# Banded attention and two gated layers on one core: a head pair's scores and products with v issued in one run per tile of tokens

## The reference

```python
scores = q @ k.T / sqrt(D)                     # float32, per batch and head
mask = (rel >= 0) & (rel < 64)                 # rel = row - column
attn = softmax(where(mask, scores, -1e9))      # sum + 1e-9 below the line
x = (attn @ v) as (2304, 512)
x = max(x @ w1, x @ w2, x @ w3) @ w_out        # 512 -> 768 -> 512
h = x @ w_in                                   # 512 -> 2048
g = where(h >= 1, h, where(h <= -1, 0, (h + 1)**2 / 4))
out = g @ w_out2                               # 2048 -> 512
```

## Time and profile before

| what | us |
|---|---|
| three runs: median, lowest, highest | 772.2, 771.97, 772.84 |
| the profiled execution: its time | 771.65 |
| its span in the trace | 769.9 |
| TensorE busy | 752.1 (98%) |
| VectorE, ScalarE, GpSimd busy | 330.5, 334.0, 312.8 |
| DMA: bytes moved, mean | 46.18 MB, 60 GB/s |

### The profile page before, as it was taken

How to read it: one execution, slowest core, us unless ns; L and a number is a source line. 1 busy time by engine, 2 the same in 40 slices (tenths; PEclk the granted TensorE clock), 3 DMA queues, 4 the chain that set the end, 5 groups by cost and what they waited for, 6 DMA issues and landing times.

```text
span 769.9 us, 12651 instructions
## 1 busy us (share of the span) xinstructions
PE 752.1 (98%) x4680; PEld 655.0 (85%) x4680; DVE 330.5 (43%) x759; ACT 334.0 (43%) x809; POOL 312.8 (41%) x242
## 2 busy tenths in 40 slices
PE   5999999999999999999999899999999999999998
PEld 3888777777787888999999798899899899899886
DVE  3363233233223202261334663565766375367334
ACT  5662533542353120354253563365555355345332
POOL 4760111210111070185235873384777266257321
PEclk9999999999999999999999999999999999999999
DMA  8633232132110210020001110001120002201302
GB/s 311 234 103 95 62 96 80 34 101 71 43 43 14 83 56 1 0 80 29 0 1 56 55 47 36 1 29 55 55 83 28 1 1 90 76 0 55 110 1 83
DMA packets 24040, 46.18 MB, mean 60 GB/s; under 512 B 2224, under 2 KB 3632, under 8 KB 23984
## 3 DMA queue, kind: packets, MB, share of 16 engines
q1 hardware_dynamic: 23984, 45.43, 17.7%
HBM read 37.55 MB, written 7.86 MB: 59 GB/s over the span
## 4 chain that ended last, share of the span: by engine, by line
PE 94%; DVE 2%; POOL 1%; ACT 1%; DMA 1%; issue 1%; SPq 0%; DVEq 0%
PE wide L523 30%; PE wide L595 25%; PE bank L575 23%; PE wide L548 8%; PE bank L509 3%; PE wide L487 3%; PE bank L498 2%; POOL w3s L990 1%; DVE part_in L938 0%; DMA q<-q_dram 0%; DMA raw<-w_dram 0%; ACT prob L617 0%; DVE h1s L812 0%; POOL prob L998 0%; ACT pT L631 0%
## 5 line engine op out<-in xcount | busy, mean ns | idle before, releaser
L523 PE MATMUL wide<-xT,w 128*128 128x512 f32 (+1 forms) x1080 | 240.5, 376 | 0.0
L523 PEld LDWEIGHTS wide<-xT,w 128*128 128x128 f32 x1080 | 186.6, 190 | 36.6 <-issue 3.4
L595 PE MATMUL wide<-w4s,gT 128*128 128x512 f32 x864 | 210.1, 392 | 0.0
L575 PE MATMUL bank<-yT,w3s 128*128 128x384 f32 x1008 | 188.2, 337 | 2.2 <-POOL w3s L990 2.2
L595 PEld LDWEIGHTS wide<-w4s,gT 128*128 128x128 f32 x864 | 161.1, 188 | 31.2
L575 PEld LDWEIGHTS bank<-yT,w3s 128*128 128x128 f32 x1008 | 178.2, 188 | 8.4 <-POOL w3s L990 2.6
L990 POOL TENSOR_TENSOR gT<-g,gT 128x384 fp32r<-128x384 f32 x96 | 105.4, 1109 | 178.4 <-ACT gT L612 178.4
L998 POOL TENSOR_TENSOR prob<-prob,row_inv 128x512 f32<-128x512 f32 x36 | 38.2, 1060 | 186.7 <-DVE row_inv L829 186.7
L735 ACT ACTIVATE g_sq<-g_sq,half 128x384 f32<-128x384 f32 x96 | 58.0, 615 | 126.9 <-DVE g_sq L925 126.6
L913 DVE TENSOR_TENSOR pu<-bank,pu 128x384 f32<-128x384 f32 x72 | 40.1, 557 | 141.5 <-PE bank L575 136.5
L843 DVE TENSOR_TENSOR h<-wide,h 128x512 f32<-128x512 f32 (+1 forms) x60 | 38.2, 637 | 104.0 <-PE wide L523 103.4
(11 more groups left out here) (52 smaller groups left out, 538.7 us busy)
## 6 DMA issues: line engine op xcount, KB each, us to landing
v<-v_dram SPq DMA_DIRECT2D x36, 256.0 KB, 2.6
raw<-w_dram SPq DMA_DIRECT2D x16, 512.0 KB, 3.5
k<-k_dram SPq DMA_DIRECT2D x16, 288.0 KB, 3.2
h<-moe_w_dram SPq DMA_DIRECT2D x12, 384.0 KB, 8.0
q<-q_dram SPq DMA_DIRECT2D x16, 256.0 KB, 3.8
part_dram<-o_sb SPq DMA_DIRECT2D x12, 256.0 KB, 2.1
part_in<-part_dram SPq DMA_DIRECT2D x2, 1536.0 KB, 7.2
out_dram<-part_in SPq DMA_DIRECT2D x11, 256.0 KB, 2.1
```

The lines of the kernel that those rows point to most:

```text
L523: mm = pe.matmul(acc[gr % 2][:, 0:cols], w123[:, wp, w, kc, c * P:(c + 1) * P], xT[:, x_side(t), xp, kc, 0:cols], start=(kc == x == 0), st ...
L575: mm = pe.matmul(bank[:, 0:MTOK], w3s[j % HALF_F][:, wp, W_OF[m], kc * P:(kc + 1) * P], yT[:, m, yp, kc, :], start=(m in (0, 1, 3) and kc ...
L595: mm = pe.matmul(acc4[b], gT[:, k, gp, tb * P:(tb + 1) * P], w4s[pair_f(g) % HALF_F][:, wp, f, :], start=(first and x == 0), stop=(last an ...
```

## The change

Scores and products with v are issued for a whole pair at once: `score(n)` makes 32 multiplications for pairs of two steps, into the two banks that its two steps share, and waits for the maxima of pair n-2; `values(n)` waits for both copies and both v and fills the whole bank of 512 columns; `x_hi` and `x_lo` are written once per pair. Maxima, exponentials, normalizing and transposes stay per step. In the order, scores stand right behind the products of the pair one or two before (`LEAD`). `prob`, `pT` and the sums get 4 places, v gets 6. All orders are new: among them the start, where SP loads v1 ahead of k2 and w1 and v0 ahead of k3, and w8 to w11 behind v10 and v11. ScalarE issues the loads of the mask, k1 and q1, ahead of everything else that it does.

```diff
+V_BUFS = 6
+PROBS = 4
...
     "SP": """
-        k0 q0 mask0 k1 q1 v0 k2 q2 v1 k3 q3 v2 v3 k4 q4 w0 w1 w2 w3 k5 q5 k6 q6 w4 w5 w6 v4 w7 k7 q7
-        v5 v6 w8 w9 v7 w10 w11 v8 v9 v10
+        k0 q0 k1 mask0 q1 v1 k2 q3 q2 v3 w1 v0 k3 w3 v2 w2 w0 k4 q4 k5 q5 w4 w5 w6 w7 k6 q6 k7 q7 v4 v5 v6
+        v7 k8 q8 v8 v9 v10 v11 w8 w9 w10 w11 k9 q9 v12 v13 k10 q10
     """,
     "PE": """
-        score0 score1 score2 probs0 score3 probs1 values0 probs2 values1 values2 probs3 values3 score4
-        score5 group0 score6 group1 group2 probs4 score7 group3 probs5 score8 group4 values4 group5 probs6
-        score9 group6 values5 probs7 score10 group7 values6 group8 probs8
+        score0 score1 score2 probs0 score3 values0 probs1 values1 probs2 values2 probs3 values3 score4
+        score5 group0 group1 group2 probs4 group3 group4 probs5 group5 values4 score6 group6 probs6 group7
+        probs7 group8 values5 score7 group9 probs8 group10 group11
     """,
     "ACT": """
-        exp0 safe0 exp1 safe1 p0 exp2 safe2 p1 exp3 x_hi0 safe3 p2 x_hi1 w_hi3 x_hi2 p3 x_hi3 exp4 group0
-        safe4 exp5 group1 safe5 w_hi7 group2 p4 exp6 group3 safe6 p5 exp7 group4 safe7 w_hi9 x_hi4 group5
-        p6 exp8 safe8 x_hi5 exp9 p7 safe9 x_hi6
+        exp0 safe0 exp1 safe1 p0 exp2 safe2 x_hi0 p1 exp3 x_hi1 safe3 p2 w_hi0 x_hi2 p3 x_hi3 w_hi5 exp4
+        safe4 group0 exp5 group1 safe5 group2 exp6 p4 group3 exp7 p5 group4 safe6 group5 safe7 x_hi4 exp8
+        p6 safe8 exp9 p7 w_hi9 safe9 w_hi10 x_hi5 w_hi11 exp10 p8 safe10 exp11
     """,
     "DVE": """
-        max0 max1 invert0 invert1 max2 invert2 max3 w_lo0 x_lo0 invert3 x_lo1
-        w_lo3 x_lo2 x_lo3 max4 w_lo4 max5 invert4 invert5 max6 max7 invert6 invert7 w_lo9 max8 x_lo4
-        group6 invert8 max9 x_lo5 w_lo8 invert9
+        max0 max1 invert0 max2 invert1 w_lo1 invert2 max3 x_lo0 w_lo3 x_lo1 invert3 x_lo2 x_lo3 max4 w_lo5
+        max5 invert4 max6 max7 invert5 w_lo7 invert6 invert7 x_lo4 max8 group6 max9 invert8 group7 group8
+        w_lo8 invert9 max10 x_lo5 group9 max11 group10 w_lo11
     """,
     "POOL": """
-        norm0 norm1 norm2 w_hi0 w_hi1 w_hi2 norm3 w_lo1 w_lo2 w_hi4 w_hi6 norm4 w_lo6 norm5 w_hi5 w_lo5
-        norm6 w_lo7 norm7 w_hi10 w_hi11 norm8 w_hi8 w_lo10 w_lo11
+        norm0 w_hi1 norm1 w_hi3 norm2 w_hi2 norm3 w_lo0 w_lo2 w_hi4 w_lo4 norm4 w_hi6 norm5 w_hi7 w_lo6
+        norm6 norm7 norm8 w_hi8 w_lo9 norm9 w_lo10
     """,
 }
+
+LOADED_BY_ACT = "mask0 k1 q1"
...
-SPREAD = {1: (3.29, 1.41), 2: (3.29, 1.15), 3: (3.8, 2.15), 4: (3.13, 0.8)}
-LAG = {1: (3.14, 1.28), 2: (3.06, 1.06), 3: (5.02, 2.19), 4: (5.79, 1.67)}
+SPREAD = {1: (3.1, 0.92), 2: (3.84, 1.35), 3: (3.93, 2.3), 4: (0.41, 2.66)}
+LEAD = {1: 2, 2: 1, 3: 2, 4: 2}
+LAG = {1: (1.26, 0.62), 2: (2.06, 0.98), 3: (3.84, 1.26), 4: (2.9, 1.73)}
...
+OF_PAIRS = ("k", "q", "score", "values", "x_hi", "x_lo")
...
+def spot(n):
+
+    a, u = divmod(n, PAIRS)
+    if a == 0:
+        return float(n - PAIRS)
     first, last = SPREAD[a]
-    values = LAYER1_AT[a - 1] + first + (length - last - first) * (PIECES[a] * u + part) / (PAIRS * PIECES[a] - 1)
-    return {"score": values - LAG[a][0], "probs": values - LAG[a][1], "values": values}
+    return LAYER1_AT[a - 1] + first + (GROUPS * GROUP[a - 1] - last - first) * u / (PAIRS - 1)
+
+
+def place(kind, i, near):
+
+    n, part = (i, 0) if kind in OF_PAIRS else (PAIR_OF[i], STEP[i][2])
+    if near == "score":
+        return spot(n - LEAD[n // PAIRS]) + STEP_APART * part
+    return spot(n) - (LAG[n // PAIRS][part] if near == "probs" else 0)
...
-    v2, at = place("v2", [P, BUFS, NB, P], F32, at)
-    prob, at = place("prob", [P, 2, NB, SPAN], F32, at)
-    pT, at = place("pT", [P, 2, NB * P], F32, at)
+    v2, at = place("v2", [P, V_BUFS, NB, P], F32, at)
+    prob, at = place("prob", [P, PROBS, NB, SPAN], F32, at)
+    pT, at = place("pT", [P, PROBS, NB * P], F32, at)
...
-    def x_of(s, part):
-
-        a, u, piece = STEP[s]
-        return xT[:, x_side(a), part, u, piece * TOK:(piece + 1) * TOK]
+    def x_of(n, part):
+
+        a, u = divmod(n, PAIRS)
+        return xT[:, x_side(a), part, u, 0:TOKENS[a]]
...
+    def load(eng, kind, i):
+
+        if kind in ("k", "q"):
+            a, u = divmod(i, PAIRS)
+            start, cols = TOK * FIRST_PIECE[a], TOKENS[a]
+            if i >= BUFS:
+                eng.wait_ge(scored, i - BUFS + 1)
+            if kind == "k":
+                eng.dma_start(k2[:, i % BUFS, 0:WINDOW + cols], k_dram[:, u, start:start + WINDOW + cols]).then_inc(k_in[i % BUFS], 16)
+            else:
+                eng.dma_start(q2[:, i % BUFS, 0:cols], q_dram[:, u, start:start + cols]).then_inc(q_in[i % BUFS], 16)
+        elif kind == "v":
+            a, u, part = STEP[i]
+            if i >= V_BUFS:
+                eng.wait_ge(valued, PAIR_OF[i - V_BUFS] + 1)
+            eng.dma_start(v2[:, i % V_BUFS, :, :].rearrange("p j n -> p (j n)"),
+                          v[(FIRST_PIECE[a] + part) * PAIRS + u, :, :]).then_inc(v_in[i % V_BUFS], 16)
+        elif kind == "mask":
+            eng.dma_start(mask[:, :, :].rearrange("p x n -> p (x n)"), masks[:, :]).then_inc(mask_in, 16)
+        else:
+            n, kc = divmod(i, KC)
+            eng.dma_start(w_stage(n, kc), w_dram[n][:, kc, :]).then_inc(w_in[i], 16)
...
+            if (kind, i) not in words_of(LOADED_BY_ACT):
+                load(sp, kind, i)
...
-        def score(s):
-            a, u, part = STEP[s]
-            n = PAIRS * a + u
-            if part == 0:
-                pe.wait_ge(q_in[n % BUFS], 16 * (n // BUFS + 1))
-                pe.wait_ge(k_in[n % BUFS], 16 * (n // BUFS + 1))
-            after(pe, maxed, NB * (s - 1))
-            for b in range(NB):
+        def score(n):
+            pe.wait_ge(q_in[n % BUFS], 16 * (n // BUFS + 1))
+            pe.wait_ge(k_in[n % BUFS], 16 * (n // BUFS + 1))
+            if n >= 2:
+                pe.wait_ge(maxed, NB * steps_of(n - 2)[1])
+            for b in range(TOKENS[n // PAIRS] // BLK):
 
                 for h in range(2):
-                    at = (NB * part + b) * BLK
-                    mm = pe.matmul(scores_in[s % 2][half_of(b % 2), h, b // 2 * SPAN:(b // 2 + 1) * SPAN],
-                                   q2[half_of(h), n % BUFS, at:at + BLK], k2[half_of(h), n % BUFS, at:at + SPAN],
+                    at = b // 2 * SPAN
+                    mm = pe.matmul(scores_in[n % 2][half_of(b % 2), h, at:at + SPAN],
+                                   q2[half_of(h), n % BUFS, b * BLK:(b + 1) * BLK], k2[half_of(h), n % BUFS, b * BLK:b * BLK + SPAN],
                                    start=True, stop=True, skip_group_check=True)
             mm.then_inc(scored, 1)
...
-                mm = pe.transpose(p_in[:, i * P:(i + 1) * P], prob[:, s % 2, i, :], ident[:, :])
+                mm = pe.transpose(p_in[:, i * P:(i + 1) * P], prob[:, s % PROBS, i, :], ident[:, :])
...
-        def values(s):
-            pe.wait_ge(v_in[s % BUFS], 16 * (s // BUFS + 1))
-            pe.wait_ge(p_copied, s + 1)
-            after(pe, x_lo, s)
-            for b in range(NB):
-
-                for h in range(2):
-                    at = (b // 2 * 2 + h) * P + b % 2 * BLK
-                    mm = pe.matmul(o_ps[half_of(h), b * BLK:(b + 1) * BLK], v2[:, s % BUFS, b, half_of(h)],
-                                   pT[:, s % 2, at:at + BLK], start=True, stop=True, skip_group_check=True)
+        def values(n):
+            first, end = steps_of(n)
+            for s in range(first, end):
+                pe.wait_ge(v_in[s % V_BUFS], 16 * (s // V_BUFS + 1))
+            pe.wait_ge(p_copied, end)
+            after(pe, x_lo, n)
+            for s in range(first, end):
+                for b in range(NB):
+
+                    for h in range(2):
+                        to = ((s - first) * NB + b) * BLK
+                        at = (b // 2 * 2 + h) * P + b % 2 * BLK
+                        mm = pe.matmul(o_ps[half_of(h), to:to + BLK], v2[:, s % V_BUFS, b, half_of(h)],
+                                       pT[:, s % PROBS, at:at + BLK], start=True, stop=True, skip_group_check=True)
             mm.then_inc(valued, 1)
...
-                    pe.wait_ge(x_lo, step_at(t, kc + 1, 0))
+                    pe.wait_ge(x_lo, PAIRS * t + kc + 1)
...
-            after(act, inverted, s - 1)
-            act.activation(safe[:, s % 2, :], row_sum[:, s % 2, :], ACT.Identity, bias=tiny[:, 0:1]).then_inc(sum_safe, 1)
+            after(act, inverted, s - PROBS + 1)
+            act.activation(safe[:, s % PROBS, :], row_sum[:, s % PROBS, :], ACT.Identity, bias=tiny[:, 0:1]).then_inc(sum_safe, 1)
...
-            after(act, valued, s - 1)
-            act.activation(pT[:, s % 2, :], p_in[:, :], ACT.Copy).then_inc(p_copied, 1)
-
-        def x_hi_of(s):
-            act.wait_ge(valued, s + 1)
-            hi(x_of(s, 0), o_ps).then_inc(x_hi, 1)
+            if s >= PROBS:
+                act.wait_ge(valued, PAIR_OF[s - PROBS] + 1)
```

(68 more changed lines are left out.)

53 lines of the change are left out of this document (9 added, 44 removed).

## The result

The changed kernel takes 758.62 us in the median (757.73 to 759.03), the kernel before in the same comparison 772.52 (771.97 to 772.89): a ratio of 0.9818, interval 0.9804 to 0.9833. The profiled execution took 757.73 us, the lowest of the four, and its span is 755.9; against the 771.65 us of the one before that is 13.9 us less, where 12.6 were forecast. The forecast of 759.6 is 1.0 us too high and its range, 757.0 to 769.0, holds the result.

What follows compares the result with a forecast made beforehand. TensorE's issue was taken as the bound, DMA rings second in the first 25.36 us alone. From span 769.9, -8.4 - 4.8 + 0.1 + 0.5 = -12.6 gives 757.3, time 759.1, median 759.6 us; range 757 to 769.

Steps and rivals of the forecast that it cites:

- The prices of the runs: TensorE's breaks between groups: 32 scores 1.03 us, 32 products 1.10, transposes alone 0.49, entering a break 0.20.
- The middle that I took for the products: Second 16 products with v in a merged run: 0.49 us, the middle between 0.43 and 0.55.
- From group 18 on: TensorE's breaks from group 18 to the end of layer 1: 38.4 us instead of 46.7, gain 8.4.
- Between groups 0 and 18: The small-group stretch: 39.3 us instead of 44.06, gain 4.8 if nothing new waits.
- the 0.5 for waits of products 4 and 5: Among small groups, values 4 and 5 may wait for their copy behind a later step's exponentials; 0.5 us put in.
- rival A: Small waits in most pairs, as two steps enter VectorE and ScalarE together: 0.5 us in 16 pairs, 767; chance 0.18.
- The start: Everything before group 0: group 0 at 25.5 us instead of 25.36, with 24.0 and 27.0 as bounds.
- k3 late for score 3: Before group 0: k3, issued behind v3, w1 and v0, comes 3 us later; score 3 waits about half a microsecond.
- After 312.94 nothing is changed: From the end of layer 1 to the end of the kernel: the same time as before.
- SP's queue: w8 to w11 behind v10 and v11, there by about 46 us, wanted in group 12 from 51.7: cost 0, little over.
- Rival C: TensorE's instructions run out inside the 64-long breaks of products with scores: 1.75 us in each of 13, 782; chance 0.09.
- My argument against the 62 ns from the old trace: Densest old break, 36 multiplications in 1.63 us, 45 ns each, speaks against a bare 62 ns per MATMUL.

Runs made afterwards that it cites:

- e3: Changed kernel with the scores of pairs 6 to 19 issued in two runs of 16, the first one group earlier; 762.23 us.
- e4: Changed kernel with the products with v of pairs 4 to 19 issued in two runs of 16, the first one group earlier; 762.64 us.
- e5: Changed kernel with both scores and products with v split into two runs; 763.44 us.
- e1: Changed kernel with SP issuing the loads of mask, k1 and q1 too, instead of ScalarE; 758.74 us.
- e12: The changed kernel itself, unchanged, run again as control; 758.08 us.
- e2: Changed kernel with scores of pairs 6 to 19 issued one group earlier, behind transposes instead of products, in runs of the same length; 759.49 us.
- e7: Changed kernel with 4 places for v again instead of 6; 765.04 us.
- e11: Changed kernel with 4 places for v and SP issuing w8 to w11 ahead of v10 and v11; 758.38 us.
- e9: Changed kernel with 40 extra calls multiplying the identity by itself in TensorE's waits before group 0; 757.15 us.
- e10: Changed kernel with 19 extra calls multiplying the identity by itself in TensorE's waits before group 0; 754.97 us.

## Why the prediction was right, point by point

- **The prices of the runs** held: 32 scores 1.04 for 1.03, 32 products 1.08 for 1.10, transposes alone 0.49. The middle that I took for the products (0.49, between 0.43 and 0.55) was a little high: it measures 0.46 to 0.47. From group 18 on the gain is 9.2 us (243.36 to 234.12) instead of 8.4. The products' middle is 0.3 of that difference, and two pairs' scores in one run 0.15 (1.91 us for 2 x 1.03); the rest is within the rounding of the prices. e3, e4 and e5 show that the merging brings 7.9 us from group 0 to layer 2. The gain by fewer breaks, which the forecast's sum holds too, was counted and not tested.
- **Between groups 0 and 18** 6.3 us instead of 4.8 less 0.5. The term that was off is the clock: I kept 1.4 us for a slow group 0, and it was not slow. And the 0.5 for waits of products 4 and 5 did not come (rival A): TensorE's busy time there equals the stretch.
- **The start**: 24.63, forecast 25.5 within 24.0 and 27.0, but not by my walk. I had the first score unmoved, and it came 1.2 us later, as the mask's, k1's and q1's loads shared the rings with k0 and q0 from the first moment (k0 landed 3.1 us after its issue, in e1 2.3); I had k3 late for score 3, and with the loads on ScalarE it was not (in e1, without them, it was, by 1.31 us). My 1.0 MB ahead of k3 was too much as well: v0 stood ahead of k3 before too, and what is new there is q3, v3 and w1, 0.79 MB, 2.4 us at the same 331 GB/s. I had all of the stretch at the lower clock, and 3.4 us of it was not. So the start came out inside its range by luck: a later first score and a partly faster clock cancelled. The clock's share is what swings most: group 0 stands at 24.21 to 25.29 us in the six profiles whose start is the same program (changed, e12, e2 to e5), and at 22.43 and 21.70 in e7 and e11, which differ from it ahead of group 0 only in when v4 to v7 may be loaded.
- **"After 312.94 nothing is changed"** is right of the program and missed 2.3 us of this execution. 1.5 of them lie ahead of the last multiplication. TensorE waits 2.25 us for GpSimd's weights' parts at 410.9, as before; in this execution the clock fell right behind it, and the next 18 multiplications took 5.5 us instead of 3.9 (429.35 to 433.27 in the trace of before):

```profile
413.20 1.95 PE L590 MATMUL bank<-yT,w3s 128*128 128x384 f32 x6 [2.25 <-POOL w3s L1010]
414.95 3.89 PE L610 MATMUL wide<-w4s,gT 128*128 128x512 f32 x12
418.67 1.57 PE L590 MATMUL bank<-yT,w3s 128*128 128x384 f32 x8
...
413.50:417.10 3.60, 3.60 (x12) 3.13 (x11) 2.35 (x4) 1.91 (x4) 0.93 (x1) 0.53 0.48 148
```

The clock fell there in 9 of the 12 profiles of the changed kernel and its variants, whose program is the same from layer 2 on. In e4, e5 and e7 it did not, and layer 2 to the start of the last multiplication took 453.4 us instead of 454.8, about the 453.25 of before. So it comes and goes with a program that is the same; whether the change makes it likelier is not shown, as there is one profile of the kernel before. The other 0.8 us lie behind the start of the last multiplication: 4.64 us against 3.83, and 4.45 to 4.69 in all twelve profiles, so these do not come and go. SP issues its last two stores in 0.64 us each in the changed kernel's profile instead of 0.41 and 0.45; why is not shown.
- **SP's queue**: I called w8 to w11 behind v10 and v11 free "with little over". It was free, and e7 shows how little: 5.7 us later in the queue cost 7.3 of standstill. I had looked at group 12, which uses these weights; TensorE would have stopped at group 11, for a drain queued behind them.
- **Rival C** is refuted for the long breaks (96 multiplications at 31 ns each). My argument against the 62 ns from the old trace was weaker than it looked: counted by calls, the densest old break was 20 calls in 1.63 us, 81 ns each, which such a limit would have allowed. The 54 ns a call in the changed kernel is what speaks against it.

## What to carry to other kernels

When TensorE is the bound, runs of small multiplications cost more than their pieces: here a run's two ends were 0.16 us and entering a break between groups 0.20. Runs of twice the length, half as many, in 32 breaks instead of 45, took 9 of 47 us from group 18 on, and not one multiplication was left out. Price a new order by start-to-start distances of each form of break in the old trace; that came within 1 us of 38. And in strictly ordered queues ask not who uses a late load but what stands behind the instruction that waits for it.

## What the runs showed of the hardware that I had not expected

A start with many short waits swings with the clock. 19 calls of otherwise useless TensorE work in such waits went with a time 3.1 us lower (ranges apart), of which the trace places 1.3 at the start, where the granted clock rose at 13.1 us and was up through group 0. Of 40 such calls less came (0.9796 of the kernel before against 0.9767, intervals that just overlap): the first twelve held up the first scores by 2.3 us.

In e11's profiled execution TensorE stands still for 2.52 us inside group 0, after 7 of its multiplications, with no semaphore as the cause. The rings are full there (20 to 26 us), and the one packet of the instruction queue q8 in that stretch starts just as TensorE stops, at 22.8 us:

```profile
21.70 1.10 PE L538 MATMUL wide<-xT,w 128*128 128x256 f32 x7
25.32 5.23 PE L538 MATMUL wide<-xT,w 128*128 128x256 f32 x29 [2.52 <-issue]
...
q1 hardware_dynamic: 1224, 2.30, 103.6%
q8 instruction: 1, 0.02, 1.1%
```

That could be instructions that came late, behind loads, at a place where 64 scores at the full clock had used them up fast: rival C's mechanism at another place. e7 has a gap of 0.15 us at the same multiplication. Against it, e9 and e10 run the same 64 scores at the full clock and have no gap in group 0, and the packet itself took about 1 us of the 2.52. It was not tested, and stays a guess.
